# Two attention-side edits in one: v loaded in 64-channel pieces and turned before the norms' steps, and the first 512 columns of w_in multiplied in three rounded passes

## What is computed

```
qn = q / (norm(q, axis=tokens) + 1e-06);  kn = likewise for k
s = kn.T @ qn / tau;  s = s - s.max(-1)            # 256 x 256
a = exp(s);  a /= a.sum(-1) + 1e-09
x = v @ a                                          # 6016 x 256
h = x @ w_in1;   g = h - tanh(h);          x = g @ w_out1
h = x @ w_in2;   g = h if h > 0 else exp(h) - 1;   out = g @ w_out2
```

## Time and profile before

| what | value |
|---|---|
| median of 3 runs | 1030.95 us (1030.77 to 1031.65) |
| the profiled execution | 1030.58 us |
| its span | 1028.8 us |
| TensorE matmul busy | 1023.7 us |
| VectorE busy | 821.3 us |
| ScalarE busy | 767.2 us |
| GpSimd busy | 0.8 us |
| mean granted TensorE clock | 0.999 |

### The profile page before, as it was taken

The page is one execution under the profiler, slowest core; times in us unless marked ns, Lnnn a source line. Parts: engine busy times, 40 slices in busy tenths (PEclk is TensorE's granted clock), DMA queues, the critical chain, the costliest instruction groups (busy, mean ns, idle before and its releaser), DMA issues.

```text
span 1028.8 us, 13741 instructions
## 1 busy us (share of the span) xinstructions
PE 1023.7 (100%) x4574; PEld 858.6 (83%) x4574; DVE 821.3 (80%) x1362; ACT 767.2 (75%) x1360; POOL 0.8 (0%) x7
## 2 busy tenths in 40 slices
PE   9999999999999999999999999999999999999998
PEld 8868888888888888888998888888888888888997
DVE  5899977777867776777999888887887887887876
ACT  6687776666766666767778878778778787878775
POOL 0000000000000000000000000000000000000000
PEclk9999999999999999999999999999999999999999
DMA  9932002003003001012212002102101201200202
GB/s 354 302 70 41 1 31 52 1 22 62 1 9 70 0 1 42 1 41 72 62 54 96 1 1 62 21 1 56 26 1 42 42 1 37 42 1 1 41 1 36
DMA packets 117830, 46.24 MB, mean 45 GB/s; under 512 B 100352, under 2 KB 108544, under 8 KB 117760
## 3 DMA queue, kind: packets, MB, share of 16 engines
q1 hardware_dynamic: 113616, 43.99, 16.0%
q10 hardware_dynamic: 4144, 1.38, 0.5%
HBM read 33.03 MB, written 12.32 MB: 44 GB/s over the span
## 4 chain that ended last, share of the span: by engine, by line
PE 98%; DVE 1%; issue 0%; DMA 0%; ACT 0%; POOL 0%; DVEq 0%; POOLq 0%
PE r_ps L327 16%; PE r_ps L326 16%; PE r_ps L328 16%; PE x_ps L327 6%; PE x_ps L328 6%; PE x_ps L326 6%; PE z_ps L328 4%; PE z_ps L327 4%; PE z_ps L326 4%; PE y_ps L327 2%; PE q_ps L327 2%; PE y_ps L328 2%; PE q_ps L326 2%; PE q_ps L328 2%; PE y_ps L326 2%; PE x_ps L333 2%
## 5 line engine op out<-in xcount | busy, mean ns | idle before, releaser
L606 ACT ACTIVATE g_hi<-g 128x512 fp32r<-128x512 f32 (+1 forms) x384 | 236.2, 616 | 137.4 <-DVE g L854 54.7
L707 DVE TENSOR_TENSOR g_lo<-g,g_hi 128x512 fp32r<-128x512 f32 (+1 forms) x384 | 259.6, 677 | 49.6 <-ACT g_hi L606 40.8
L326 PE MATMUL r_ps<-g_hi,w_out_hi 128*128 128x512 f32 (+1 forms) x768 | 296.1, 385 | 0.0
L328 PE MATMUL r_ps<-g_hi,w_out_lo 128*128 128x512 f32 (+1 forms) x768 | 295.7, 385 | 0.0
L327 PE MATMUL r_ps<-g_lo,w_out_hi 128*128 128x512 f32 (+1 forms) x768 | 295.7, 385 | 0.0
L326 PEld LDWEIGHTS r_ps<-g_hi,w_out_hi 128*128 128x128 f32 x768 | 144.2, 188 | 27.5 <-DVE g_lo L707 0.6
L328 PEld LDWEIGHTS r_ps<-g_hi,w_out_lo 128*128 128x128 f32 x768 | 144.2, 188 | 26.8
L327 PEld LDWEIGHTS r_ps<-g_lo,w_out_hi 128*128 128x128 f32 x768 | 144.2, 188 | 26.6
L326 PE MATMUL x_ps<-t_hi,w_ops 128*128 128x512 f32 (+1 forms) x288 | 111.4, 387 | 0.0
L327 PE MATMUL x_ps<-t_lo,w_ops 128*128 128x512 f32 (+1 forms) x288 | 111.0, 385 | 0.0
L328 PE MATMUL x_ps<-t_hi,w_ops 128*128 128x512 f32 (+1 forms) x288 | 110.9, 385 | 0.0
(11 more groups left out here) (109 smaller groups left out, 1485.0 us busy)
## 6 DMA issues: line engine op xcount, KB each, us to landing
v_blocks<-v_dram SPq DMA_DIRECT2D x40, 128.0 KB, 3.0
x_scratch<-side SPq DMA_DIRECT2D x20, 256.0 KB, 2.0
vt<-x_scratch SPq DMA_DIRECT2D x20, 256.0 KB, 3.5
out_dram<-v_blocks SPq DMA_DIRECT2D x80, 64.0 KB, 1.9
k_ring<-k_dram SPq DMA_DIRECT2D x9, 512.0 KB, 10.1
q_ring<-q_dram SPq DMA_DIRECT2D x9, 512.0 KB, 10.9
w_out_raw<-moe_w_out_dram SPq DMA_DIRECT2D x1, 2048.0 KB, 15.2
w_raw<-moe_w_in_dram SPq DMA_DIRECT2D x16, 128.0 KB, 2.5
```

What stands on the lines that cost most here:

```text
L326: nc.tensor.matmul(ps, w_hi, m_hi, start=start, stop=False, skip_group_check=True)
L328: return nc.tensor.matmul(ps, w_lo, m_hi, start=False, stop=stop, skip_group_check=True)
L606: nc.scalar.activation(g_hi[b][n % DEPTH[b]][:, 0:width], g[b][:, 0:width], ACT.Copy).then_inc(g_rounded[b], 1)
L707: return nc.vector.tensor_tensor(lo, x, hi.bitcast(F32), ALU.subtract)
```

## The change

v is loaded with four transfers of 32 x 32 runs of 64 channels for each pair of tiles, where there were eight with runs of 32 channels. The tile `v_pieces` holds them, and `transpose_v` reads every second channel of it. So channel 2s + i of a row takes the place that i*128 + s had, and k's columns are read in the same order (`k_channels`). Two of the four first transposes move ahead of the wait on the square root, and two go ahead of the wait on the copied norms.

The parts of the fold with gg = 0 (n = 0 and n = 2) take three float32r passes. For this ScalarE rounds the first 512 columns of w_in1 (`round_w_in`, 128x512 twice) and GpSimd forms the remainder; ScalarE rounds each half of the transposed exponential (`round_aT`) and VectorE forms its remainder (`split_aT`). The float32 copy `copy_aT`, which the other groups need, stays, and now waits for `split_aT`.

```
+IN_THREE = 1
             def load_v(p):
...
-                for block in range(C // BLOCK):
-                    cc, b = divmod(block, P // BLOCK)
-                    channel = block * BLOCK
-                    sp.dma_start(v_blocks[b * BLOCK:(b + 1) * BLOCK, cc, 0:n].rearrange("i (e c) -> i e c", c=BLOCK),
-                                 rows[:, :, channel:channel + BLOCK]).then_inc(loaded_v, 16)
+                for b in range(P // BLOCK):
+                    sp.dma_start(v_pieces[b * BLOCK:(b + 1) * BLOCK, 0:n // BLOCK, :],
+                                 rows[:, :, b * PIECE:(b + 1) * PIECE]).then_inc(loaded_v, 16)
...
+            for i in range(IN_THREE):
+                group = slice(i * 512, (i + 1) * 512)
+                for d in range(CC):
+                    pool.wait_ge(w_in_rounded, CC * i + d + 1)
+                    nc.gpsimd.tensor_tensor(w_in_lo[:, d, group], w_in1_sb[:, d, group],
+                                            w_in_hi[:, d, group].bitcast(F32), ALU.subtract).then_inc(w_in_split, 1)
...
+        def k_channels(rows, m):
+            return rows.rearrange("p (i s) -> p s i", s=CC)[:, m, :]
...
-                    last = nc.tensor.matmul(scores_ps[m][:, 0:C], k_ring[i % RING][:, r, m * P:(m + 1) * P],
+                    last = nc.tensor.matmul(scores_ps[m][:, 0:C], k_channels(k_ring[i % RING][:, r, :], m),
...
             def wf_product(n, rows=range(CC)):
-                pe.wait_ge(aT_ready, m + 1)
+                pe.wait_ge(aT_rounded, m + 1)
...
+                if gg < IN_THREE:
+                    columns_of, rows_of = slice(gg * 512, (gg + 1) * 512), slice(m * P, (m + 1) * P)
+                    pe.wait_ge(w_in_split, CC * (gg + 1))
+                    for d in rows:
+                        nc.tensor.matmul(wf_ps[n][:, :], aT_hi[:, d, rows_of], w_in_hi[:, d, columns_of], start=d == 0, stop=False,
+                                         skip_group_check=True)
+                        nc.tensor.matmul(wf_ps[n][:, :], aT_hi[:, d, rows_of], w_in_lo[:, d, columns_of],
+                                         start=False, stop=False, skip_group_check=True)
+                    pe.wait_ge(aT_split, m + 1)
+                    for d in rows:
+                        last = nc.tensor.matmul(wf_ps[n][:, :], aT_lo[:, d, rows_of], w_in_hi[:, d, columns_of],
+                                                start=False, stop=d == CC - 1, skip_group_check=True)
...
+            def round_w_in(i):
+                act.wait_ge(loaded_w_in1_first[i], 16)
+                group = slice(i * 512, (i + 1) * 512)
+                for d in range(CC):
+                    nc.scalar.activation(w_in_hi[:, d, group], w_in1_sb[:, d, group], ACT.Copy).then_inc(w_in_rounded, 1)
+
+            round_w_in(0)
             act.wait_ge(norms_ready, 1)
             nc.scalar.activation(root, norms_ps[:, 0:2 * CC], ACT.Sqrt).then_inc(rooted, 1)
...
             def copy_aT(m):
-                act.wait_ge(prob_transposed, m + 1)
+                act.wait_ge(aT_split, m + 1)
...
             norm_steps = [0]
+            transpose_v(0, 0, 0)
+            transpose_v(0, 0, 1)
             dve.wait_ge(rooted, 1)
```

More of the change, by code:

```diff
@@ L123, in attention_ffn_kernel @@
             w_in1_sb = sb("w_in1_sb", [P, CC, F], stack=early)
+        with ExitStack() as early:
+            w_in_lo = sb("w_in_lo", [P, CC, F], F32R, early)
             w_out_raw = sb("w_out_raw", [P, UNITS, C], stack=early)
@@ L133, in attention_ffn_kernel @@
             aT = sb("aT", [P, CC, C], stack=early)
+            aT_hi, aT_lo = sb("aT_hi", [P, CC, C], F32R, early), sb("aT_lo", [P, CC, C], F32R, early)
+            w_in_hi = sb("w_in_hi", [P, CC, IN_THREE * 512], F32R, early)
         t_hi, t_lo = [None, None], [None, None]
@@ L136, in attention_ffn_kernel @@
             t_hi[b], t_lo[b] = sb(f"t_hi{b}", [P, OPS, TILE], F32R), sb(f"t_lo{b}", [P, OPS, TILE], F32R)
+        with ExitStack() as early:
+            v_pieces = sb("v_pieces", [P, 2 * TILE // BLOCK, PIECE], stack=early)
         v_blocks = sb("v_blocks", [P, CC, 2 * TILE])
@@ L168, in attention_ffn_kernel @@
         loaded_tau, loaded_v, loaded_w_in1, loaded_w_out1 = sem("loaded_tau"), sem("loaded_v"), sem("loaded_w_in1"), sem("loaded_w_out1")
-        loaded_w_in1_first = sem("loaded_w_in1_first")
+        loaded_w_in1_first = [sem(f"loaded_w_in1_first{i}") for i in range(IN_THREE)]
+        w_in_rounded, w_in_split = sem("w_in_rounded"), sem("w_in_split")
+        aT_rounded, aT_split = sem("aT_rounded"), sem("aT_split")
         loaded_w_in2 = [sem(f"loaded_w_in2_{i}") for i in range(QUADS)]
@@ L353, in _ @@
                     for col, (acc, m) in enumerate(((q_acc, 0), (q_acc, 1), (k_acc, 0), (k_acc, 1))):
-                        last = nc.tensor.matmul(norms_ps[:, col:col + 1], acc[:, 0, m * P:(m + 1) * P], ones[:, 0:1],
+                        channels = acc[:, 0, m * P:(m + 1) * P] if acc is q_acc else k_channels(acc[:, 0, :], m)
+                        last = nc.tensor.matmul(norms_ps[:, col:col + 1], channels, ones[:, 0:1],
                                                 start=col == 0, stop=True, skip_group_check=True)
@@ L382, in wf_product @@
                     pe.wait_ge(wf_copied, n - 5)
+                if gg < IN_THREE:
[10 more added lines that the diff above has]
+                                                start=False, stop=d == CC - 1, skip_group_check=True)
+                    last.then_inc(wf_multiplied, 1)
+                    return
+                pe.wait_ge(aT_ready, m + 1)
                 for d in rows:
@@ L560, in _ @@
             round_t(0, P1)
+            round_aT(0)
+            round_t(0, P2)
             copy_aT(0)
-            round_t(0, P2)
             exp_scores(1)
             round_t(0, P5)
+            round_aT(1)
             copy_aT(1)
@@ L819, in scale_scores, with split_aT @@
                 nc.vector.tensor_reduce(neg_max[:, m:m + 1], prob[:, m, :], AX.X, ALU.max, negate=True).then_inc(max_ready, 1)
+            def split_aT(m):
+                dve.wait_ge(aT_rounded, m + 1)
+                rows_of = slice(m * P, (m + 1) * P)
+                minus(aT_lo[:, :, rows_of], aT_ps[m][:, 0:C].rearrange("p (d c) -> p d c", d=CC),
+                      aT_hi[:, :, rows_of]).then_inc(aT_split, 1)
             def invert_sum(m):
@@ L838, in _ @@
             form_t(0, P6)
+            split_aT(1)
             invert_sum(1)
```

33 lines of the change are left out of this document (21 added, 12 removed).

## The result

The changed kernel takes **1038.19 us** (median of 4 runs, 1037.49 to 1039.26) beside 1030.86 (1030.71 to 1031.65) for the kernel before: a ratio of 1.0072, 95% interval 1.006 to 1.0084. Slower was forecast, with 1034.6 us and a range up to 1037.6. It came out 3.6 us later than that, 0.6 outside the range.

The account below looks back on a forecast made before the run. TensorE, holding 98% of the chain, was taken as the bound. A 2.9 us stop plus 0.9 at the first split weights, less 0.1, gave +3.7: 1034.6 us against the median of 1030.95, range 1031.8 to 1037.6.

Parts of the forecast that it names:

- the stop: TensorE's wait for the diagonal behind the norms: predicted to stand still for 2.9 us.
- Part 2: Rounding w_in ahead of ScalarE's square root: w_in lands at 43.2, the root begins at 44.4, 3.2 us late.
- upper bound: v's 256-byte runs at 24 ns each, twice the 128-byte price; v then lands at 40.3 to 41.0.
- the rival in which the rest is later: Slower 256-byte runs, v in at 40.3 to 41.0 and w_in at 44.8: +5.3, 1036.3 us; chance 0.08.
- Part 3: v's early transposes on VectorE: first pair ends at 41.0 ahead of the root, second fits before the scaling; no cost.
- Parts 4 and 5: Second exponential turned 0.2 us earlier, 0.1 in the sum; first split weights 0.9 us later, behind the second aT remainder.
- Part 1: TensorE's fold: six float32r passes for two float32 matmuls save 0.7 us over two parts, showing nowhere in the sum.
- Part 6: The rest: GpSimd's two remainders have 6.6 us, over 3 us each, before aT is rounded; no cost taken.
- The clock in the stop: Rival: TensorE's stop ahead of the diagonal sends the clock to half: +2.9 us, 1037.5; chance 0.10.
- Strided weight loads: k's weights read with step two: priced at zero; rival that loads outgrow the matmul, up to +33 us, chance 0.04.

Follow-up runs that it names:

- e10: Changed kernel with w_in's first columns loaded ahead of v, GpSimd held until the diagonal, transposes between later steps, copy_wf(0) and copy_wf(1) ahead of copy_aT(1): 1030.75 us.
- e1: Changed kernel with GpSimd's two remainders held back until the diagonal is ready: 1036.68 us, ratio 1.0052.
- e2: Changed kernel with nine unneeded matmuls of ones in TensorE's list ahead of its wait for the diagonal: 1037.2 us, ratio 1.0063.
- e5: Changed kernel with 18 unneeded matmuls of ones in TensorE's list ahead of its wait for the diagonal: 1035.93 us, ratio 1.0044.
- e3: Changed kernel with the two roundings of w_in1 moved behind the square root and table load on ScalarE: 1032.8 us, ratio 1.0029.
- e8: Kernel before with v's pieces of 64 channels, k's strided reads and the four early transposes, fold left in float32: 1032.11 us, ratio 1.0011.
- e9: Kernel before with v's pieces of 64 channels and k's strided reads, transposes at their old places: 1031.22 us, ratio 1.0002.
- e4: e3 with copy_wf(0) and copy_wf(1) moved ahead of copy_aT(1) on ScalarE: 1035.92 us, ratio 1.0045.
- e7: e3 with GpSimd held until the diagonal, transposes between the later steps, and copy_wf(0) and copy_wf(1) ahead of copy_aT(1): 1032.47 us, ratio 1.0008.
- e12: e10 without the hold on GpSimd, which takes its remainders as soon as w_in is rounded: 1035.06 us, ratio 1.0032.
- e11: Changed kernel with v in runs of 128 bytes, k read as before and transposes at their old places: 1040.77 us, ratio 1.0093.

## Why the prediction was right and wrong

The forecast added 3.7 us and 7.8 came: 1.2 more in the stop (4.14 for 2.9, of which GpSimd's 1.1 is the failed step), 2.8 from the clock, which the sum left out, and nothing in the rest. This split is that of one execution.

*Part 2, the rounding ahead of the root: the mechanism right, the number by luck.* Root at 44.53, predicted 44.4. But errors cancelled in it. I priced 256-byte runs at 17 ns; 37 to 40 moved 178 GB/s, hardly more than 128-byte runs (171), which is 256 x 16 / 178 = 23 ns, near my upper bound. w_in was issued at 37.17, not 36.4; that the queue was full, as I said, no run tests. v's transposes began at 42.45, not 39.7, which is also later than the 40.3 to 41.0 of the upper bound, and the rest of it stays open. w_in then landed 1.0 us behind v and not 3.8, so at 43.47 (predicted 43.2). I had called its slowness its own; in e10, ahead of v but behind chunks of q and k, it took 7.7 us from issue to landing, so being behind v doesn't explain it either. And e1, e2 and e5 have the root at 45.9 to 46.2, as in the rival in which the rest is later. e10 adds that w_in's place in the queue decides when it is in: at 37.5 there.

*Part 3, the transposes: right in the sum, wrong in the reason.* "The first pair can start when v is in, at 39.7, and ends at 41.0, ahead of the root": it ended at 43.8. It cost nothing only because the root was later still. e3 has the diagonal 1.6 us late for it once the root is early, and e8's median is 0.9 over e9's.

*Parts 4 and 5, the second exponential and the first split weights: right.* -0.18 and +0.99 for a predicted -0.1 and +0.9, and e4 and e7 show the cause of most of it.

*Part 1 never showed in the time*, as said. The passes are shorter as priced: from the start of the second folded part to that of the fourth TensorE took 3.10 us (56.93 to 60.03) and before 3.44 (50.15 to 53.59), 0.34 for the one rounded part in it. But even e10 doesn't have the waits at their old places. v lands late there, its transposes hold the first scaling until 45.63 (44.87 before), and TensorE waits 0.51, 0.37 and 0.32 us, more than the 0.7. Its first split product starts 0.65 us later than in the kernel before (59.29 against 58.64).

*Part 6, "That leaves 6.6 us for two, over 3 us each": wrong, the first failed step.* A remainder takes 1.26 us (2.48 for the two, which overlap a little), and GpSimd was in time. The step asked only whether it ends in time and not who suffers beside it. Its 1.1 us lie in the chain of the six steps. e1 removes them, e4 and e12 enlarge them. The Trainium skill (SBUF — State Buffer, section "SBUF: two separate sides") has the rule that I left out: VectorE and GpSimd share one pair of ports, and a VectorE instruction with two SBUF inputs (against a GpSimd instruction that reads SBUF), or in a mode that uses both ports, is fully blocked until the GpSimd instruction that holds the pair is over. The traces agree. GpSimd's first remainder ran from 44.18 to 45.44, and L866, begun at 44.71, ended at 45.47. The second ended at 46.66, and L869, begun at 45.92, at 46.69. L868, with an operand in PSUM, took 0.16 beside it, and in e3 two transposes beside GpSimd kept 1.30.

*The clock in the stop: wrong by its chance, the second failed step and the largest.* It was a rival at 0.10, +2.9 us, 1037.5. It happened with +2.8. Set against it was only "Before, TensorE is never idle for 2.9 us", and that says nothing about what such a stop does. e5 isolates it. That the size fits is luck: from the diagonal to the turning of the first exponential it takes 3.15 us at full clock (e3, e5), and 4.76 in e1, 4.83 in e4, 5.26 in e11, 6.05 in the changed kernel and 6.10 in e2. So the lower clock took 1.6, 1.7, 2.1, 2.9 and 3.0 us, behind stops of 3.79, 2.24, 6.57, 4.04 and 2.74. Add the 1.1 of GpSimd to this rival's 1037.5, and the forecast is 1038.6, 0.4 from the result.

*Strided weight loads: right* (e9).

## What to carry to other kernels

When TensorE is the belt, price a stop at a wait as its own length and again as what the halved clock may take behind it: here 4 us of stop cost 2.8 more, and stops of 2.2 to 6.6 us in the other runs 1.6 to 3.0, not in the order of their length. Before work is handed to an idle GpSimd, list VectorE's SBUF-only instructions in the same microseconds; each may be held until a GpSimd instruction ends, however small it is (0.76 us for 0.17 and 2.54 for 0.48 here, while the reciprocal of 128x4 kept 0.18 and a pair of transposes 1.30). And if an engine is made to wait for a transfer in front of its critical instruction, move the transfer forward in the queue before moving the work: e10 did the same fold at no cost that could be measured.

## What the runs showed of the hardware that was not expected

- VectorE beside a GpSimd subtraction of 128x512: 0.17 to 0.76 us for 128x4, 0.42 to 1.48 for 128x256, 0.69 to 1.46 for an addition of 128x512, 0.48 to 2.54 for two diagonals. GpSimd too took longer, 2.98 for its two instructions in e12 and 2.48 to 2.52 elsewhere.
- The clock read 1.00 behind stops of 1.04 us (e3) and 0.67 (e5) and was lower behind 2.24 (e4), 2.69 (e12), 2.74 (e2), 3.79 (e1), 4.04 and 6.57 (e11). But e8 has it at 0.57 in 43 to 47, behind a stop of 1.28 ahead of the norms, and e4 at 1.00 in 43 to 47, behind one of 1.93 at the same place. So the length of the stop alone doesn't separate these cases, and what does stays open.
- Runs of 256 bytes moved v at 178 GB/s in 37 to 40 (148 to 193 in the same stretch of e1 to e10), runs of 128 bytes at 171: half the descriptors gave no faster landing.
